# Attention and two MLPs on one Trainium2 core: 512-token tiles and attention in 128-token steps in the first stage, inputs laid out head-dimension first, weights split in place

## The reference

```
# q, k, v: (8 batches, 8 heads, 576 tokens, 64), float32
k_p = k.reshape(B, H, 72, 8, 64).mean(axis=3)           # keys averaged over 8 tokens
v_p = v.reshape(B, H, 72, 8, 64).mean(axis=3)
scores = q @ k_p.T / sqrt(64);  attn = softmax(scores)   # with 1e-9 added to the sum
x = (attn @ v_p), heads side by side: (4608, 512)
h = max(x @ w1, x @ w2, x @ w3)                          # 512 -> 768
x2 = h @ w_out                                           # 768 -> 512
u = x2 @ w_in                                            # 512 -> 2048
out = (u - tanh(u)) @ w_out2                             # 2048 -> 512
```

## Time and profile before

| | us |
|---|---|
| median of three runs (1603.13 to 1604.36) | 1603.88 |
| profiled execution: first to last instruction | 1601.1 |
| what lies around the span, by these two | 2.8 |
| PE busy | 1555.5 (97%) |
| DVE, ACT, POOL busy | 999.5, 600.0, 70.9 |

### The profile page before, as it was taken

One profiled execution on the slowest core, in us unless ns is written; L12 is line 12 of the kernel. 1 busy time (PEld: TensorE's weight loads), 2 busy tenths in 40 slices (PEclk: granted clock), 3 DMA queues, 4 the chain that ended last, 5 costly groups with the idle time before them and its releaser, 6 DMA issues.

```text
span 1601.1 us, 25315 instructions
## 1 busy us (share of the span) xinstructions
PE 1555.5 (97%) x9824; PEld 1402.6 (88%) x9824; DVE 999.5 (62%) x1604; ACT 600.0 (37%) x1119; POOL 70.9 (4%) x38
## 2 busy tenths in 40 slices
PE   3999999999999999999988999999999999999999
PEld 3899999999999999999977888888888888888887
DVE  6776464646647465433377667667667676676766
ACT  3423333223232332232354444443444444444433
POOL 2500000000000000002022000000000000000000
PEclk9999999999999999999999999999999999999999
DMA  8441122211122222001230101000000001010000
GB/s 205 116 113 40 32 56 59 59 49 42 42 49 54 54 64 68 9 20 57 79 109 1 53 1 53 0 28 26 26 26 26 27 14 39 0 53 1 27 1 27
DMA packets 70197, 72.22 MB, mean 45 GB/s; under 512 B 40016, under 2 KB 48208, under 8 KB 70128
## 3 DMA queue, kind: packets, MB, share of 16 engines
q1 hardware_dynamic: 66384, 56.63, 12.8%
q0 software_dynamic: 3744, 14.68, 2.8%
HBM read 52.43 MB, written 18.87 MB: 45 GB/s over the span
## 4 chain that ended last, share of the span: by engine, by line
PE 90%; DVE 6%; ACT 1%; issue 1%; DMA 1%; SPq 0%; DVEq 0%; ACTq 0%
PE psum L527 27%; PE psum L596 24%; PE psum L582 23%; PE psum L541 9%; PE psum L473 2%; PE psum L497 2%; PE psum L483 2%; DMA v_raw<-in_v 1%; PE psum L460 1%; DVE k_pooled L841 1%; DVE g L966 1%; DVE v_sum L841 0%; DVE probs L861 0%; DVE row_sum L877 0%; DVE poly L977 0%
## 5 line engine op out<-in xcount | busy, mean ns | idle before, releaser
L527 PE MATMUL psum<-x,w 128*128 128x288 f32 x3456 | 475.6, 297 | 1.6 <-DVE x L870 1.2
L527 PEld LDWEIGHTS psum<-x,w 128*128 128x128 f32 x3456 | 463.1, 189 | 5.0 <-DVE x L870 1.4
L596 PE MATMUL psum<-w_out_s,g 128*128 128x512 f32 x1728 | 418.9, 392 | 10.3 <-DVE g L966 10.3
L596 PEld LDWEIGHTS psum<-w_out_s,g 128*128 128x128 f32 x1728 | 326.6, 189 | 80.1 <-DVE g L966 11.9
L977 DVE SCALAR_TENSOR_TENSOR poly<-poly,u_sq 128x512 f32<-128x512 f32 x144 | 102.1, 709 | 236.7 <-ACT poly L791 236.7
L783 ACT ACTIVATE u_sq<-psum 128x512 f32<-128x512 f32 x144 | 86.1, 598 | 427.2 <-PE psum L582 427.2
L582 PE MATMUL psum<-x_even,w_in_s 128*128 128x512 f32 x960 | 230.0, 389 | 0.0
L582 PEld LDWEIGHTS psum<-x_even,w_in_s 128*128 128x128 f32 x960 | 180.1, 188 | 37.5
L582 PE MATMUL psum<-x_odd,w_in_s 128*128 128x512 f32 x768 | 184.5, 389 | 0.0
L582 PEld LDWEIGHTS psum<-x_odd,w_in_s 128*128 128x128 f32 x768 | 144.1, 188 | 29.9
L541 PE MATMUL psum<-h,w_mid_s 128*128 128x288 f32 x1152 | 160.8, 297 | 0.0
(11 more groups left out here) (60 smaller groups left out, 1107.1 us busy)
## 6 DMA issues: line engine op xcount, KB each, us to landing
q_raw<-in_q SPq DMA_DIRECT2D x48, 192.0 KB, 2.8
x_scratch<-x_stage SPq DMA_DIRECT2D x64, 144.0 KB, 1.8
x_raw<-x_scratch SPq DMA_DIRECT2D x9, 1024.0 KB, 5.2
out<-out_stage SPq DMA_DIRECT2D x36, 256.0 KB, 2.1
v_raw<-in_v SPq DMA_DIRECT2D x15, 576.0 KB
k_raw<-in_k SPq DMA_DIRECT2D x14, 576.0 KB
stage_a<-in_moe_w POOLq DMA_DIRECT2D x6, 768.0 KB, 6.7
stage_b<-in_moe_w_out POOLq DMA_DIRECT2D x4, 1024.0 KB, 6.6
```

The costliest lines, as they stand in the source:

```text
L527: mm = pe.matmul(psum[:, bank, 0:NH], w123[:, ws, n, c, m * P:(m + 1) * P], x[:, xs, c, h * NH:(h + 1) * NH], start=(c == 0 and ws + xs == ...
L596: mm = pe.matmul(psum[:, j, :], g[:, m % 4, gs, j * P:(j + 1) * P], w_out_s[:, m // 4, ws, m % 4, :], start=(m == 0 and gs + ws == 0), sto ...
```

## The change

- **Layout of the inputs.** The inputs are rearranged on the host before the launch. q arrives as pairs of heads by tokens (`(4, 128, 4608)`), so that a load puts it head dimension first into `q_t`, ready as a matmul operand; PE's transposes of q and ACT's copies of them are gone. k arrives head dimension first too, with the 8 tokens of a mean side by side: its sum lies as PE wants it, and the transposes of the keys are gone. v has the 8 tokens side by side. The division by 8 of the values moves into the softmax's denominator (L740 of the new kernel), and ACT's scaling copy of the values is gone.
- **First MLP on 512-token tiles**, nine of them, across the batches. Layer 1 has blocks of 36 matmuls with 512 columns, layer 2 has 18 with 512. In tile 0 layer 1 is cut in two halves of 256 tokens, all six blocks for the first half and then all six for the second.
- **Attention in 36 steps of 128 tokens.** Steps 4, 13, 22 and 31 hold tokens of two batches: their scores are 8 matmuls with 64 stationary columns and their product with the values is 16 matmuls with 64 moving columns. The scores, transposes and products are entries of their own (`score`, `turn`, `attend`, `norm`), ahead of the MLP by one tile.
- **Order.** `make_order` builds one list for the whole of stage 1, with no loop. After an `l1` entry comes directly `h1`, its split. The reductions of the next batch (4 for k and 4 for v, a pair behind a block) are taken from a list of waiting work.
- **Weights split in place.** A piece is loaded over the place of its own low part; ACT writes the high part beside it and POOL overwrites the raw values with the low part. The staging buffers are gone. All loads are issued by SP. There are 20 pieces: 6 of w1, w2 and w3 (one block of 128 output channels of all three matrices each), 2 of w_mid, 6 of w_out and 6 of w_in (three chunks each, the last one). Eight are split at the start, nine during the last tile of stage 1, and three (`IN_TILE_0`) behind chunks 2, 3 and 4 of stage 2. x2 is also split in place, in two buffers, and the load for tile t+2 waits until PE has finished `hidden` of tile t.

The core of the diff:

```diff
+STEPS = TOKENS // P
+HALF = TB // 2
+QSLOTS = 4
+PIECES = [("w123", m) for m in range(MC1)] + [("mid", 0), ("mid", 1)] + [
+    ("out", 0), ("in", 0), ("out", 1), ("in", 1), ("out", 2), ("in", 2), ("in", 3), ("in", 4), ("in", 5),
+    ("out", 3), ("out", 4), ("out", 5)]
+IN_TILE_0 = [("out", 3), ("out", 4), ("out", 5)]
...
+    for m in range(MC1):
+        l1(0, m, 0, HALF)
+        slot(*[[("split", 2), ("score", 2), ("norm", 2)],
+               [("split", 3), ("turn", 2), ("score", 3), ("norm", 3)],
+               [("split", 4), ("attend", 2), ("turn", 3)],
+               [("split", 5), ("attend", 3)],
+               [("split", 6)], [("split", 7)]][m])
+
+    for t in range(NT):
+        a = 4 * t + 4
+        more = t < NT - 1
+        after_l1 = [[("score", a), ("norm", a)], [("turn", a)], [("attend", a), ("score", a + 1), ("norm", a + 1)],
+                    [("turn", a + 1)], [("attend", a + 1), ("score", a + 2), ("norm", a + 2)],
+                    [("turn", a + 2), ("score", a + 3), ("norm", a + 3)]]
+        after_l2 = [[("attend", a + 2), ("turn", a + 3)], [("attend", a + 3)], [], []]
...
+        for m in range(MC1):
+            l1(t, m, HALF if t == 0 else 0, TB)
+            slot(*after_l1[m])
+        for c in range(KC1):
+            then(("l2", t, c))
+            slot(*after_l2[c])
...
+            load_q(0)
+            for p in range(PAIRS):
+                sp.dma_start(k_first[:, p].rearrange("p n t -> p (n t)"), k[0, p]).then_inc(k_first_in[p], 16)
...
+            load_q(1)
+            load_piece(0)
+            load_q(2)
+            load_piece(1)
+            load_q(3)
+            for i in range(2, MC1 + 2):
+                load_piece(i)
+                if i in (3, 4):
+                    load_k(1, i - 3)
+                    load_v(1, i - 3)
...
+            for i in range(len(PIECES)):
+                _, raw, hi, lo = piece(i)
+                pool.wait_ge(piece_hi, i + 1)
+                nc.gpsimd.tensor_tensor(lo, raw, as_f32(hi), ALU.subtract).then_inc(piece_ready, 1)
...
+            def score(n):
+                pe.wait_ge(q_in[n % QSLOTS], 16 * (n // QSLOTS) + 16)
+                pe.wait_ge(k_ready, parts_of(n)[-1][2] + 1)
...
+                    for row, rows, b in parts_of(n):
+                        mm = pe.matmul(psum[row:row + rows, 4 + pr // 2, (pr % 2) * 2 * KEYS:(pr % 2 + 1) * 2 * KEYS],
+                                       q_t[:, n % QSLOTS, pr, row:row + rows], k_diag[:, b % 2, pr, :],
+                                       start=True, stop=True)
...
-                            mm = pe.matmul(psum[:, bank, 0:NH], w123[:, ws, n, c, m * P:(m + 1) * P],
-                                           x[:, xs, c, h * NH:(h + 1) * NH],
...
+                            mm = pe.matmul(psum[:, bank, 0:hi - lo], w123[:, m, ws, n, c, :],
+                                           x[t % 2][:, xs, c, lo:hi],
...
+                nc.vector.tensor_scalar(row_eps[:], row_sum[:], 1e-9, float(POOL), ALU.add, ALU.mult)\
+                    .then_inc(softmax_step, 1)
...
+        "q": q.reshape(B, PAIRS, 2, S, D).transpose(1, 2, 4, 0, 3).reshape(PAIRS, P, TOKENS),
...
+        "k": k.reshape(B, PAIRS, 2, S, D).transpose(0, 1, 2, 4, 3).reshape(B, PAIRS, P, S),
...
+        "v": v.reshape(B, H, KEYS, POOL, D).transpose(0, 2, 1, 4, 3).reshape(B, KEYS, DM * POOL),
```

985 lines of the change are left out of this document (412 added, 573 removed), and 5 rows, old and new, of the table ORDER.

## The result

The changed kernel takes 1554.21 us (median of four runs, 1553.13 to 1557.35) against 1604.12 us before (four runs, 1603.13 to 1604.50). The ratio is 0.9695, with a 95% interval of 0.9681 to 0.9709, so it is 3% faster. The forecast was 1544.6 us with a range of 1520 to 1568. The profiled execution took 1554.3 us with a span of 1552.5 us, 10.7 us more than the 1541.8 us of the sum. Most of this part is about where those 10.7 us went. One of the four executions of `e9_pad128` further down took 2063.95 us at a granted clock of 0.695 and is left out of the comparisons.

The account below looks back on a forecast made before the run. PE bounds the kernel, busy 1555.5 of 1601.1 us. Sum: 1601.1 - 23.0 (matmuls) - 33.3 (attention) + 3 (start) - 6 (change of stage) = 1541.8 us, plus 2.8 us of median over span: 1544.6 us, range 1520 to 1568.

Parts of the forecast that it names:

- Matmuls, -23.0 us: MLP layers 1 and 2: same columns in fewer, wider matmuls, 12.7 ns fixed each, 590.3 us against 613.3.
- Attention, -33.3 us: Stage 1 attention on PE: 36 steps instead of 48, no transposes of q or keys, 110.6 us against 143.9.
- the seams: Stage 1 attention: extra PE time put at 0.5 us a tile, 4.5 us in the sum.
- The rest of attention hidden, the 0.7 us margin: Softmax on DVE and ACT costs nothing behind MLP blocks; tightest at a tile's fourth step, ready 6.3 us, asked 7.0.
- second rival (late softmax): Fourth step's margin gone, transposes wait some 2 us in each of nine tiles: 1563 us, chance 9%.
- The start, +3 us: Kernel start through tile 0: first block at 37 us, 45 us lost against 41.9; bounds -12 to +16.
- the two meetings of POOL and DVE: At the start, POOL's first two weight splits fall on the two `norm` entries, costing 3 us each.
- The last tile, nothing: Stage 1's last tile: nine weight splits beside 8.16 us blocks cost nothing; uncovered, each up to 3.5 less 1 us.
- The change of stage, -6 us: Start of stage 2: fewer POOL subtractions, PE loses 8.5 us instead of 14.5; bounds -11.5 to +0.5.
- the smaller stop: After the change of stage: a smaller PE stop expected besides one like before, together 8.5 us.
- cheap start: Rival at the start: POOL and DVE do not meet, keys come in time, PE loses 32 us: 1532 us, 12%.
- DVE waits for keys and values: Rival in each batch: late loads hold DVE, 3 us in 28 slots gives 1629 us; decides from 2.2; slower 3%.

Follow-up runs that it names:

- e9_pad128: Changed kernel with 128 more instructions without effect (waits on a set semaphore) at PE's very start, stage 2's loop kept; 1552.08 us, ratio 0.9678.
- e1_narrow: Changed kernel with every 512-column matmul of layer 1 made as two of 256 columns; 1564.47 us, ratio 0.9755 to the kernel before.
- e2_turn_q: Changed kernel with four float32 transposes of 128 columns put back ahead of each step's scores, results unused; 1561.87 us, ratio 0.9733.
- e6_whole_tile0: Changed kernel with tile 0 not halved, four attention steps first, splits of pieces 4 to 7 behind the blocks; 1546.72 us, ratio 0.9648.
- e3_pool_waits: Changed kernel with POOL's first two low parts of weights held until the first and second softmax are done; 1549.72 us, ratio 0.9662.
- e5_late_split: Changed kernel with stage 2's three weight splits behind chunks 5, 7 and 8 instead of 2, 3 and 4; 1552.63 us, ratio 0.9691.
- e7_x2_early: Changed kernel with the x2 split for stage 2's first tile one block earlier in stage 1's last tile; 1550.56 us, ratio 0.9670.
- e10_before_pad220: Kernel before, with PE's program moved by 220 more instructions (waits on a set semaphore) ahead of its work; 1612.9 us, one execution.

## Why the prediction was right, and where 10.7 us were missed

- **Matmuls, -23.0 us**: right. The block takes 8.16 us, and the fixed cost is 12.2 to 12.4 ns by `e1_narrow` where 12.7 was used. (The rows of before leave 13.1 and 13.3 ns over N/2.4 for the two shapes, not 13.3 for both; nothing in the sum uses it.)
- **Attention, -33.3 us**: right in mechanism, some 2 us too much. From tile 1 to stage 2, 612.6 us less 8 x 288 x 226.7 ns (522.3) less 2.0 of the stop leave 88.3 us for 28 steps; the forecast's prices give 28 x 2.88 + 3 x 0.6 + 8 x 0.5 = 86.4. On average the scores took 0.93 us (priced 0.98), the transposes 0.82 (0.93) and the product 1.02 (0.97), 0.1 us less a step than forecast, and the steps with two batches 0.1 to 0.2 us more for each of two pieces, not 0.6. The term that was mis-sized is the seams: a block behind a change of shape takes up to 0.2 us more, about 1.4 us in each tile with attention where 0.5 was put. `e2_turn_q` puts back the transposes of q; what 36 steps save against 48 is read from the pieces, and no run puts them back.
- **The rest of attention hidden, the 0.7 us margin**: right. The second rival (late softmax) did not occur in any full tile.
- **The start, +3 us**: the mechanism is right and was paid as forecast, 3.3 and 3.0 us for the two meetings of POOL and DVE. The first block came at 38.54 us (37), the end of the six half blocks at about 80.5 (77; the 72 matmuls from 76.11 to 84.91 us are the sixth and the first of the second half), and the second halves lost the 5 us they were given (59.8 us to tile 1, for 54.7 of work). Tile 1 began at 140.33 us, where the forecast's terms give 51.71 (layer 1 of tile 0) + 16.32 (its layer 2) + 24.14 (eight steps) + 45 (lost) = 137.2. That is 3.1 us; with the start's other outcome it would have been 136.0, so which side of the forecast it fell on was decided by less than 0.4 us.
- **The last tile, nothing**: wrong by 2.0 us. The forecast named a price for a lost cover, up to 3.5 us less 1 us of slack, and did not put it in the sum. Each split by itself is covered; two in a row with the split of x2 beside them are not. I had costed the nine one by one and had not laid them beside DVE's other work of that block.
- **The change of stage, -6 us**: one stop of 3.50 us and one slow block of 1.9 us over, 5.4 us, where 8.5 were put. Here the forecast was too dear by 3.1 us, since the smaller stop did not come.
- **What was not in the sum**: the stops at the jumps back, 4.5 us of standing and some 1.5 of a lower clock behind the second (start to start, the two blocks take 5.00 and 6.97 us for 2.72, 6.5 us too much). Stage 2 takes 792.7 to 792.9 us in the four kernels whose loop is kept and has no such stop (`e1_narrow`, `e2_turn_q`, `e6_whole_tile0`, `e9_pad128`), and 799.1 to 799.8 in the changed kernel, `e3_pool_waits`, `e5_late_split` and `e7_x2_early`: 6.8 us for the changed kernel against `e9_pad128`. This is the step that failed: I took stage 2's loop, 730 us without a gap in the earlier trace rows, as unchanged, because the work in it is.

Together: +3.1 (start) + 1.9 (attention) + 2.0 (last tile) + 3.6 (stage 2: 799.6 against 783.5 + 8.5 + 4) = 10.6 of the 10.7 us. That the errors of single terms partly offset each other (3.1 us too dear at the change of stage, 6.8 us for the stops that nobody counted) is luck.

The rival *cheap start* (1532 us) did not happen; `e3_pool_waits` makes half of it by hand, and it is worth 5.7 us at the first block, not 13. The rival *DVE waits for keys and values* happened in small: in the steady part DVE waits for loads eight times, 11.7 us for values and 2.5 for keys, up to 4.8 us at once (375.36 us). It does not reach PE, which stands for 1.8 us in all there, and not at those places. (Its threshold of 2.2 us a slot is 2.1 by the forecast's own numbers, 59.3 us in 28 slots.)

## What to carry to other kernels

- A place where two engines lock each other out has a length, and it is that of the instruction that holds the lock. Cut the holder's instructions short before moving work about: here one such edit of three lines gave 10.5 us (some 4 of them are the start's other outcome), and moving the same work later gave nothing in its stage.
- Read a change by stretches, not by its total. Three edits moved PE's program without meaning to, and that was worth 6.8 us in a place that they did not touch; on totals alone, each would have been misjudged. The test for it is cheap: shift the program by some instructions of no effect, and look for stops of kind `issue` behind a loop's jump back and for the packets of the instruction queue.
- "It is hidden" is to be said of a block with everything that stands in it. Two hidden pieces that meet in one block can be uncovered.

## What the runs showed of the hardware

- A DVE product with two SBUF operands that starts 10 ns after a POOL subtraction of 1536 elements takes 4.02 us instead of 0.76, and with POOL instructions of 512 elements 1.57 us. POOL's own three instructions take 4.23 us together where the single one takes 3.42.
- A loop of PE with the same instructions runs without a gap in one place of the program, and in another stands for 1.7 to 2.6 us at each jump back, with 65 packets in the instruction queue instead of 48 (`e9_pad128`), or 59 instead of 41 (`e10_before_pad220`).
- A DVE `tensor_scalar` of 8 elements with one SBUF operand, begun 40 ns behind a POOL subtraction of 1536 elements, took 3.41 us instead of 0.17 (`e2_turn_q`), and begun 0.76 us behind it 2.68 us (`e9_pad128`).
- After a stop of 3.5 us, 12 matmuls of 512 columns took 4.61 to 5.49 us, after one of 2.33 us 4.59 or 3.06, and after one of 1.38 us 3.03 (2.88 in an undisturbed stream, by the records).
